# Three reorderings in a fused attention and two-layer feed-forward kernel: `normalise` on VectorE, stores and loads on SP, and the buffers of the w2 weights

## The reference

```python
# attention in chunks of 32 queries; 8 heads, 4 batches of 768 tokens, head_dim 64
k_full = concat([mem_k (8), k[c_start-16 : c_end+8]])      # 64 keys for a chunk
scores = (q_c @ k_full.T) / 8;  a = softmax(scores);  out = a @ v_full
x = out as [3072, 512]
# first feed-forward
h = x @ w_in            # [3072, 2048]
g = h * cos(h)
y = g @ w_out           # [3072, 512]
# second feed-forward
h = max(y @ w1, y @ w2, y @ w3)      # [3072, 768]
return h @ w_out2                    # [3072, 512]
```

## Time and profile before

| what | value |
|---|---|
| median of 3 runs | 1003.52 us (1003.38 to 1003.9) |
| profiled execution, its own time | 1003.52 us |
| its span, first to last instruction | 1001.7 us |
| mean granted TensorE clock | 0.983 of 2.4 GHz |
| busy: PE, DVE, ACT, POOL | 962.1, 675.9, 516.0, 210.2 us |
| chain that ended last | PE 73%, ACT 10%, DVE 9%, DMA 4% |

### The profile page before, as it was taken

How to read it: one execution, slowest core, us unless ns; L and a number is a source line. 1 busy time by engine, 2 the same in 40 slices (tenths; PEclk the granted TensorE clock), 3 DMA queues, 4 the chain that set the end, 5 groups by cost and what they waited for, 6 DMA issues and landing times.

```text
span 1001.7 us, 18402 instructions
## 1 busy us (share of the span) xinstructions
PE 962.1 (96%) x7564; PEld 933.3 (93%) x7564; DVE 675.9 (67%) x926; ACT 516.0 (52%) x689; POOL 210.2 (21%) x231
## 2 busy tenths in 40 slices
PE   5989999999999999999999999999999999999998
PEld 4878889898989899989999999999999999999998
DVE  4355666566665568997998989866736546577761
ACT  1586786867778788333433334543323224444441
POOL 3341111112121212100100000662100000584610
PEclk6799999999999999999999999999999999999999
DMA  9983656574653434443445434432020031324532
GB/s 223 227 212 101 185 149 187 145 201 129 192 165 111 149 131 155 149 145 125 149 145 172 148 106 133 140 120 92 32 95 32 33 127 48 121 95 146 192 116 84
DMA packets 65395, 135.41 MB, mean 135 GB/s; under 512 B 5920, under 2 KB 27424, under 8 KB 65312
## 3 DMA queue, kind: packets, MB, share of 16 engines
q1 hardware_dynamic: 54944, 98.58, 34.2%
q0 software_dynamic: 10368, 35.66, 10.8%
HBM read 87.03 MB, written 47.19 MB: 134 GB/s over the span
## 4 chain that ended last, share of the span: by engine, by line
PE 73%; ACT 10%; DVE 9%; DMA 4%; issue 3%; POOL 1%; SPq 1%; DVEq 0%; ACTq 0%
PE ps L595 23%; PE ps L597 22%; PE ps L596 22%; PE ps L611 2%; DVE work L1178 2%; ACT work L901 2%; PE ps L636 2%; DVE units L1215 2%; ACT work L896 1%; ACT work L903 1%; PE ps L645 1%; DMA early_qk<-qk_in 1%; DVE ssum L1145 1%; ACT work L893 1%; ACT work L872 1%
## 5 line engine op out<-in xcount | busy, mean ns | idle before, releaser
L595 PE MATMUL ps<-units 128*128 128x384 f32 (+1 forms) x1940 | 611.1, 315 | 8.3 <-DVE units L1215 2.0
L597 PE MATMUL ps<-units 128*128 128x384 f32 (+1 forms) x1940 | 602.9, 311 | 0.0
L596 PE MATMUL ps<-units 128*128 128x384 f32 (+1 forms) x1940 | 602.6, 311 | 0.0
L595 PEld LDWEIGHTS ps<-units 128*128 128x128 f32 x1940 | 369.4, 190 | 20.2 <-issue 6.9
L596 PEld LDWEIGHTS ps<-units 128*128 128x128 f32 x1940 | 369.6, 191 | 0.0
L597 PEld LDWEIGHTS ps<-units 128*128 128x128 f32 x1940 | 369.2, 190 | 0.0
L921 ACT CAST units<-work 128x1024 fp32r<-128x1024 f32 x96 | 85.7, 939 | 123.9 <-DVE work L1201 106.6
L1076 ACT COPY work<-ps 128x384 f32<-128x384 f32 (+1 forms) x144 | 63.6, 454 | 146.9 <-PE ps L597 146.8
L1173 DVE SCALAR_TENSOR_TENSOR work<-work 128x768 f32<-128x768 f32 x64 | 62.2, 972 | 71.8 <-ACT work L896 71.8
L1215 DVE TENSOR_TENSOR units<-work,units 128x1024 fp32r<-128x1024 f32 x96 | 102.1, 1105 | 12.2 <-ACT units L921 12.2
L486 POOL DMA_DIRECT2D g_dram<-work x64 | 46.8, 731 | 291.4 <-DVE work L1178 286.7
(11 more groups left out here) (96 smaller groups left out, 845.4 us busy)
## 6 DMA issues: line engine op xcount, KB each, us to landing
g_dram<-work POOLq DMA_DIRECT2D x64, 384.0 KB, 3.3
work<-g_dram SPq DMA_DIRECT2D x48, 512.0 KB, 3.7
work<-qk_in SPq DMA_DIRECT2D x36, 384.0 KB, 5.3
work<-v_in SPq DMA_DIRECT2D x40, 256.0 KB, 5.0
work<-w_in POOLq DMA_DIRECT2D x40, 256.0 KB, 3.6
h_dram<-work SPq DMA_DIRECT2D x24, 384.0 KB, 2.9
work<-h_dram SPq DMA_DIRECT2D x18, 512.0 KB, 3.9
work<-y_dram SPq DMA_DIRECT2D x8, 768.0 KB, 6.5
```

What stands on the lines that cost most here:

```text
L595: pe.matmul(o, wh, mh, start=start, stop=False, skip_group_check=onto)
L596: pe.matmul(o, wh, ml, start=False, stop=False, skip_group_check=onto)
L597: return pe.matmul(o, wl, mh, start=False, stop=stop, skip_group_check=onto)
```

## The change

It has three parts.

VectorE, first stage: `normalise` is issued behind `turn` and `gated` of the same odd f, instead of ahead of them (in tile 0 the `shift` at f = 11 goes with it).

SP: `store_y(b-1)` stands at unit 8b instead of 8b+2, so ahead of `load_g(8b+2)` and `load_g(8b+3)`; `load_y(0)` stands at unit 24 instead of 28; `load_y` of later blocks stands ahead of the stores of the block, and no longer waits for w2; `load_h(3)` to `load_h(5)` come behind `store_hidden2(10)`, and `load_h(6)`, `load_h(7)` behind `store_hidden2(11)`.

POOL: the w2 slices go through two buffers, `raw_w` and `late`. `late` lies in slot 11 of the operands, where g of the second stage is kept, so its first load waits for the end of that stage. Each load is followed by its own sums.

```diff
-        W2_RING = (0, 0, 1, 2, 0, 1, 2, 0, 0)
+        late = plain("late", 11 * UCOLS, RAWCOLS)
+        raw_late = raw_at(late[:, :])
...
                     sp.wait_ge(y_ready, 7 * blk)
-                    sp.wait_ge(w2_ready, 7)
...
             for n in range(UNITS1):
-                if n % FPAIRS == 2 and n > 2:
+                if n % FPAIRS == 0 and n:
                     store_y(n // FPAIRS - 1)
-                if n == 3 * FPAIRS + 4:
+                if n == 3 * FPAIRS:
                     load_y(0)
                 if n >= 2 and n + 2 < UNITS1:
                     load_g(n + 2)
             store_y(NBLK1 - 1)
             for blk in range(NBLK2):
+                if blk < NBLK2 - 1:
+                    load_y(blk + 1)
                 for i in range(NPAIR):
-                    q = NPAIR * blk + i
-                    if q == GROUPS - 2:
-                        load_h(3)
-                        load_h(4)
-                    elif q == GROUPS - 1:
-                        load_h(5)
-                        load_h(6)
-                        load_h(7)
-                    store_hidden2(q)
-                    if i == 0 and blk < NBLK2 - 1:
-                        load_y(blk + 1)
-                    if q == GROUPS - 3:
-                        for r in range(NPAIR):
+                    store_hidden2(NPAIR * blk + i)
+                    if blk == NBLK2 - 1 and i < 2:
+                        for r in range(NPAIR * i, NPAIR * (i + 1)):
                             load_h(r)
...
             def load_w2(u):
                 if u == 0:
                     pool.wait_ge(w1_ready, FPAIRS)
-                elif u in (2, 3):
-                    pool.wait_ge(y_ready, 7)
+                elif u < 3:
+                    pool.wait_ge(w2_ready, u)
+                elif u == 3:
+                    pool.wait_ge(unit_done, UNITS1)
                 else:
-                    pool.wait_ge(w2_ready, {1: 1, 4: 2, 5: 3, 6: 4, 7: 5, 8: 8}[u])
+                    pool.wait_ge(w2_ready, u - 1)
...
-            load_w2(0)
-            sums_w2(0)
-            load_w2(1)
-            sums_w2(1)
-            load_w2(2)
-            load_w2(3)
-            sums_w2(2)
...
+            for u in range(UNITS):
+                load_w2(u)
+                if u != 3:
+                    sums_w2(u)
+                if u == 3:
+                    sums_w2(3)
...
-                    elif not last:
-                        if f == 2:
-                            sums(0, NSUB, NSUB + t + 1)
-                        elif f == 3:
-                            normalise(n)
-                        elif f == 7:
-                            normalise(n + 1)
-                        elif f == 11:
-                            normalise(n + 2)
+                    elif f == 2 and not last:
+                        sums(0, NSUB, NSUB + t + 1)
                     if f % 2:
                         i = FPAIRS * t + f // 2
                         turn(i)
                         if i:
                             gated(i - 1)
...
                     elif not last:
-                        if f == 4:
+                        if f == 3:
+                            normalise(n)
+                        elif f == 4:
                             x_low(n)
```

More of the change, by code:

```diff
@@ L500, in load_w2 @@
                     pool.wait_ge(w1_ready, FPAIRS)
[L501 to L505 removed]
+                elif u < 3:
+                    pool.wait_ge(w2_ready, u)
+                elif u == 3:
+                    pool.wait_ge(unit_done, UNITS1)
+                else:
+                    pool.wait_ge(w2_ready, u - 1)
+                raw, landed = (raw_late, w2_landed[1]) if u >= 3 and u % 2 else (raw_w, w2_landed[0])
                 for half in range(2):
@@ L512, in sums_w2 @@
             def sums_w2(u):
-                raw = raw_d[W2_RING[u]]
-                pool.wait_ge(w2_landed[W2_RING[u]], 32 * (W2_RING[:u].count(W2_RING[u]) + 1))
+                late = u >= 3 and u % 2
+                raw = raw_late if late else raw_w
+                pool.wait_ge(w2_landed[1] if late else w2_landed[0],
+                             32 * ((u - 1) // 2) if late else 32 * (u + 1 if u < 3 else u // 2 + 2))
                 pool.tensor_tensor(raw[:, 5, :], raw[:, 0, :], raw[:, 2, :], ALU.subtract).then_inc(w2_sums, 1)
@@ L931, in high_w2 @@
                     act.wait_ge(h_done, TILES)
-                raw = raw_d[W2_RING[u]]
+                if u == UNITS - 1:
+                    act.wait_ge(w2_ready, u)
+                raw = raw_late if u >= 3 and u % 2 else raw_w
                 act.copy(operand(s)[:, 0, :, :], raw).then_inc(w2_high, 1)
@@ L1301, in _ @@
                     if first:
-                        if f == 10:
+                        if f == 9:
+                            normalise(n)
+                        elif f == 10:
                             x_low(n)
+                        elif f == 11:
+                            normalise(n + 1)
+                            shift(n + NSUB)
                         elif f == 12:
@@ L1306, in _ @@
                             x_low(n + 1)
+                        elif f == 13:
+                            normalise(n + 2)
                         elif f == 14:
@@ L1314, in _ @@
                             shift(n + NSUB)
+                        elif f == 7:
+                            normalise(n + 1)
                         elif f == 8:
```

30 lines of the change are left out of this document (4 added, 26 removed).

## The result

The changed kernel takes 1102.33 us (median of 4 runs, 1098.09 to 1106.08), the kernel before 1003.45 on the same chip. The ratio is 1.0987, with a 95% interval from 1.0946 to 1.1028. The prediction said 1081 and a range of 1050 to 1100. So the direction and most of the size are right, and the time lies 21 us above the forecast and 2 above the range's end. The profiled execution took 1102.78 us, with a span of 1101.0.

What follows compares the result with a forecast made beforehand. The prediction took TensorE to bound the kernel, so that its waits lengthen it. Its terms, 37.2 + 17.5 + 6.6 + 6.0 + 10.4 = 77.7 us, added to 1003.52 gave 1081 us, range 1050 to 1100.

Steps and rivals of the forecast that it cites:

- Part 1: First stage: `normalise` behind `turn` and `gated` makes TensorE wait at `turn_out` in 21 places, 37.2 us.
- Part 2: Second stage: stores of y ahead of `load_g` delay g at units 10, 18, 26, 34, 42, 17.5 us.
- Part 3: Start of third stage: two w2 buffers instead of three make TensorE wait for ScalarE's snaps, 6.6 us.
- Part 4: Start of fourth stage: loads of h behind `store_hidden2` delay a cast and the snap behind it, 6.0 us.
- Part 5: Granted clock: 6.5 of eleven TensorE waits longer than 2.52 us lower it, 10.4 us, bounds 0 and 17.6.
- (a): Rival: only the first-stage waits count, VectorE's slack and earlier loads cover the queues' moves; 1047 us, chance 0.17.
- (b): Rival: the clock never falls for the new waits, which stand alone between dense matmuls; 1071 us, chance 0.17.
- (c): Third-stage rival: VectorE slows POOL's sums, 1.3 us for each of five units, every clock fall counted; 1095 us, chance 0.11.
- (d): First-stage rival: earlier `turn` and `gated` store g earlier and gain 0.61 us in 21 places; 991 us, chance 0.03.
- (e): Rival: `turn_out` is hidden by something else and the kernel stays at 1003.5 us, chance 0.02.

Runs made afterwards that it cites:

- e10: The changed kernel with identity products, results not kept, ahead of TensorE's waits in tiles 0 to 6 and at units 10, 18, 26, 34, 42: 1087.44 us.
- e6: The kernel before with `normalise` between `turn` and `gated`, half of the move: 1019.48 us, ratio 1.0155.
- e9: The kernel before with two buffers for w2 and `load_y` at the head of each block: 1015.25 us, ratio 1.0111.
- e2: The kernel before with only `store_y` ahead of `load_g` and `load_y(0)` at unit 24: 1036.01 us, ratio 1.0307.
- e3: The kernel before with only the two-buffer ring for w2, `load_y` left in place: 1012.3 us, ratio 1.0072.
- e4: The kernel before with only `load_h(3)` to `load_h(7)` behind the stores of h: 1010.37 us, ratio 1.0066.
- e5: The kernel of e1 with twelve identity products ahead of the wait at f = 4 of tiles 1 to 6: 1040.58 us, ratio 1.0367.
- e8: The kernel before with the softmax sums moved to f = 15 of the tile before (f = 5 in tile 0): 999.73 us, ratio 0.9961.
- e1: The kernel before with only VectorE's first-stage order changed, `normalise` behind `turn` and `gated`: 1051.13 us, ratio 1.0455.
- e7: The kernel of e2 with `load_y(0)` left at unit 28: 1031.89 us, ratio 1.0276.
- e12: The kernel of e8 with the sums of w1 moved to f = 7 and a tile's first `shift` to f = 8: 1011.61 us, ratio 1.0072.

## Why the time was missed, step by step

**Part 1, 37.2 us: right, in tile 0 partly by luck.** Without clock falls stage one grew by 38.7 us (e10). The waits of 1.59 at f = 8 and 12, in 6 tiles, and 3.1 at f = 4 are those forecast; in tile 0 `turn_out` came 75.14 - 69.71 = 5.4 us later, 1.9 of it start-up, so 3.5 against 3.4. But the wait there is 6.91 us, not the 5.2 forecast. Before, TensorE worked at half clock from 63.0 to 66.2, between `values` and `turn_out`; after the change it did not, was ready 1.6 us sooner and waited that much longer. The square holds `gated` back, as the earlier trace rows showed, and e6 shows that `gated` is the costly one of the two.

**Part 2, 17.5 us: right in kind, 3.2 short.** The waits are 3.81, 2.40, 8.21, 2.77 and 2.28 + 1.21 us at units 10, 18, 26, 34 and 42, together 20.7, against 3.5, 1.2, 6.1, 2.3 and 4.4. Three landings were taken too short. The `load_g` behind six stores at unit 10 went out at 494.10 and its data was there at 498.54, 4.4 us instead of 3.7. At unit 18, behind four stores, it was 538.07 to 542.99, 4.9 us, which is the whole miss of 1.2 there. That behind `load_y(0)` took 586.07 to 593.91:

```profile
584.74 1.23 SPq L357 DMA_DIRECT2D work<-y_dram  x2
586.07 12.37 SPq L334 DMA_DIRECT2D work<-g_dram  x3
```

7.8 instead of the 6.7 of the earlier trace rows, which was not behind 1.5 MB.

**Part 3, 6.6 us: right in sum.** The snaps wait 3.15, 2.17, 0.72 and 0.37 us, 6.4 together:

```profile
727.41 0.45 PE L579 MATMUL ps<-units 128*128 128x384 f32 x1 [3.15 <-ACT work L1062]
...
732.36 0.73 POOL L511 TENSOR_TENSOR late<-late 128x256 f32<-128x256 f32 x1 [6.07 <-DMA late<-w_in]
...
737.69 0.45 PE L579 MATMUL ps<-units 128*128 128x384 f32 x1 [2.17 <-ACT work L1062]
```

The second came about through the landing beside `load_y(1)`, 725.20 to 732.36, 7.2 us against 5.5 taken; the wait was still 2.17 against 2.5. "The early `load_y` for later blocks costs nothing" was wrong of the first of them (e9): that its buffer was free and its data wanted late says nothing of the transfer beside it.

**Part 4, 6.0 us: right.** 6.37 us for the second snap of the unit, and two of 0.42 and 0.48. By the prediction's reckoning 5.3 and 0.7.

**Part 5, 10.4 us: the step that failed.** It prices the clock: "I take 6.5 of them to lower it", at 1.6 us each. The 6.5 had no reason given. In the changed kernel 15 TensorE waits that the change made are 2.17 us or longer, and 14 of them had a granted clock of 0.50 in them or right behind them. The count was cut at 2.52 us, the one wait of before that had lowered it, but 2.17, 2.28 and 2.40 did so too; and by its own rule it left one out, unit 42, for which part 2 had 4.4 us. And long waits cost more than one stretch: 6.8 us at half clock around the waits of 6.91 and 6.37, 10.2 around that of 8.21. Together it is 65.1 - 6.8 = 58.3 us more at half clock. The work done in it, 47.0 us more, makes 23.5 us, against 10.4. Even the upper bound of 17.6 was low.

TensorE's busy and idle time say the same. Its busy time, for the same matmuls, grew from 962.1 to 991.0:

```profile
PE 991.0 (90%) x7564; PEld 954.5 (87%) x7564; DVE 672.2 (61%) x926; ACT 515.6 (47%) x689; POOL 197.7 (18%) x231
```

Idle it stood for 1001.7 - 962.1 = 39.6 us before and for 1101.0 - 991.0 = 110.0 after. So idle time grew by 70.4 us, where parts 1 to 4 make 67.3, and busy time by 28.9, where part 5 has 10.4. Of the 21.6 us that the span lies above the forecast, 3.1 are waits and 18.5 are longer work: 13.1 more for the clock than forecast, 1.6 for a start-up with 3.2 us more of work at half clock (8 to 39 us, which the change does not reach), and about 4 that the half-clock stretches don't account for; these stay open. Removing the half clock gave less: e10 had 65.1 - 20.5 = 44.6 us less of it and was 15.4 us faster, 0.34 for each, or 20 us for all 58.3. That is on the low side, for its waits for snaps, which were not filled, came out 3.1 us longer (16.8 against 13.7). The clock is thus worth 20 to 24 us, by either way about twice the forecast.

**The rivals.** (a), only part 1 counts, fell with e2 to e4, which cost about 45 us together. (b), the clock never falls for the new waits, is refuted by the granted clock of the changed kernel, and e5 and e10 show that the falls cost time. (c), at 1095, came nearest in time, nearer than the forecast, in part by luck. One half of it held, every clock fall counted. The other did not: a sum on POOL took up to 1.77 us beside VectorE, but the waits behind the first two of stage three are 0.72 and 0.37 us, far from 1.3 for each of five units. (d) and (e) are excluded by the result; an earlier `turn` gave nothing back.

## What to carry to other kernels

The input that the bounding engine needs next should not stand behind an instruction that waits for a third engine: put what it waits for first, and what waits itself last. When pricing a stall of TensorE, price the clock too: in the changed kernel nearly every wait of 2.17 us or longer went with half clock, about 1.6 us for each stretch of 3.4 in which TensorE works, and where waits can't be removed, products nobody keeps, put ahead of them, gave 9 to 15 us back in all. After removing a wait, look at the same engine's next one, for the work that it had covered (here the sums of w1) is now late, and moving one more item (the `shift`) too late for its own consumer lost more than all was won.

## What the runs showed of the chip

- A wait's length alone did not decide on the clock. The waits of 2.19 to 2.23 us of e6 lowered it three times in six, and one of 1.97 us at the start of stage four did so in e3, e5 and e8 but not in e1, e2, e6, e7, e9 and e12. The 2.84 us of e3 did not. In the changed kernel one wait of 2.58 us at 64.46 did not, where 2.52 did before, nor did one of 3.29 us at 378.66. Before, one stretch at half clock (441.5 to 445.5) stood behind waits of only 0.92 and 0.82 us. What separates these is open.
- A transfer was slowed by one issued just ahead of it on another queue: w2(3), 0.5 MB on GpSimd's queue, was in use 3.65 us after its issue alone (e3), 7.55 us behind 1.5 MB on SP's (e9), and 7.2 in the changed kernel.
